# Fourier filter and two gated products in fp32r on one core: a 498-column last super-tile, the second-layer weights split by GpSimd and passed through DRAM, and a reordered first and last unit

## The reference

```python
X = np.fft.rfft(x, axis=1)
y = np.fft.irfft(X * (filt_r + 1j * filt_i)[None], n=3008, axis=1)
t = y.reshape(6016, 256)
h = t @ w_in1
t = np.where(h > 0, h, np.exp(np.minimum(h, 0)) - 1) @ w_out1
h = t @ w_in2
out = (h * np.clip(h + 3, 0, 6) / 6) @ w_out2
```

## Time and profile before

| | |
|---|---|
| median of 3 runs | 1104.79 us (1104.62 to 1105.99) |
| profiled execution | 1103.63 us, span 1101.8 us, mean granted clock 0.999 |
| PE busy | 1093.9 us, 99% of the span |
| PEld, DVE, ACT, POOL busy | 882.8, 757.3, 765.9, 280.4 us |
| DMA | 54.20 MB, 49 GB/s in the mean |

### The profile page before, as it was taken

One profiled execution on the slowest core, in us unless ns is written; L12 is line 12 of the kernel. 1 busy time (PEld: TensorE's weight loads), 2 busy tenths in 40 slices (PEclk: granted clock), 3 DMA queues, 4 the chain that ended last, 5 costly groups with the idle time before them and its releaser, 6 DMA issues.

```text
span 1101.8 us, 13377 instructions
## 1 busy us (share of the span) xinstructions
PE 1093.9 (99%) x4798; PEld 882.8 (80%) x4798; DVE 757.3 (69%) x941; ACT 765.9 (70%) x1149; POOL 280.4 (25%) x215
## 2 busy tenths in 40 slices
PE   9999999999999999999999999999999999999998
PEld 4666878888888888888887888888888888888886
DVE  7998676666666676676687866665665666666665
ACT  0554788788788788888898666566666666666654
POOL 4757051111111111120398620120121021020000
PEclk9999999999999999999999999999999999999999
DMA  9755200200100101101211201001101001000001
GB/s 288 241 173 175 91 1 3 74 1 14 63 1 31 44 1 38 39 1 38 76 58 57 76 1 38 38 1 38 38 1 38 38 1 38 38 1 1 38 1 38
DMA packets 29330, 54.20 MB, mean 49 GB/s; under 512 B 3408, under 2 KB 19664, under 8 KB 29264
## 3 DMA queue, kind: packets, MB, share of 16 engines
q1 hardware_dynamic: 23648, 44.12, 12.0%
q10 hardware_dynamic: 5616, 9.22, 2.5%
HBM read 34.83 MB, written 18.51 MB: 48 GB/s over the span
## 4 chain that ended last, share of the span: by engine, by line
PE 91%; ACT 4%; DVE 2%; issue 1%; POOL 1%; ACTq 0%; POOLq 0%
PE ps L479 43%; PE ps L470 13%; PE ps L468 13%; PE ps L469 13%; PE ps L432 3%; PE ps L400 3%; PE ps L408 2%; DVE e L776 2%; PE ps L417 1%; ACT e L634 1%; ACT w_hi L606 1%; ACT e L636 1%; PE ps L419 1%; PE ps L420 1%; PE ps L438 0%
## 5 line engine op out<-in xcount | busy, mean ns | idle before, releaser
L790 DVE TENSOR_TENSOR g_lo<-e,g_hi 128x502 fp32r<-128x502 f32 (+1 forms) x288 | 276.5, 988 | 135.0 <-ACT g_hi L669 134.3
L468 PE MATMUL ps<-op_hi,w_hi 128*128 128x502 f32 x672 | 261.9, 390 | 0.0
L470 PE MATMUL ps<-op_lo,w_hi 128*128 128x502 f32 x672 | 261.8, 390 | 0.0
L469 PE MATMUL ps<-op_hi,w_lo 128*128 128x502 f32 x672 | 261.2, 389 | 0.0
L479 PE MATMUL ps<-g_lo,w_hi 128*128 128x502 f32 x766 | 236.9, 390 | 1.2 <-DVE g_lo L790 0.9
L479 PE MATMUL ps<-g_hi,w_hi 128*128 128x502 f32 x766 | 235.7, 389 | 0.2 <-ACT g_hi L669 0.2
L479 PE MATMUL ps<-g_hi,w_lo 128*128 128x502 f32 x766 | 234.9, 388 | 0.0
L873 POOL TENSOR_TENSOR op_lo<-op_raw,op_hi 128x1004 fp32r<-128x1004 f32 (+1 forms) x48 | 100.8, 2102 | 448.3 <-ACT op_hi L614 448.1
L479 PEld LDWEIGHTS ps<-g_lo,w_hi 128*128 128x128 f32 x766 | 143.3, 188 | 32.4 <-DVE g_lo L790 3.9
L479 PEld LDWEIGHTS ps<-g_hi,w_hi 128*128 128x128 f32 x766 | 143.7, 188 | 29.9 <-ACT g_hi L669 1.2
L479 PEld LDWEIGHTS ps<-g_hi,w_lo 128*128 128x128 f32 x766 | 144.1, 188 | 29.3
(11 more groups left out here) (74 smaller groups left out, 1147.9 us busy)
## 6 DMA issues: line engine op xcount, KB each, us to landing
op_raw<-y SPq DMA_DIRECT2D x36, 251.0 KB, 3.6
x_ring<-x_dev SPq DMA_DIRECT2D x32, 192.0 KB, 4.9
y<-ystage SPq DMA_DIRECT2D x12, 502.0 KB, 2.9
out_dev<-ystage SPq DMA_DIRECT2D x11, 502.0 KB, 2.9
y<-ystage ACTq DMA_DIRECT2D x18, 235.0 KB, 2.5
f_ring<-f_dev SPq DMA_DIRECT2D x11, 384.0 KB, 6.6
w_raw<-w_dev ACTq DMA_DIRECT2D x16, 256.0 KB, 4.5
w_raw<-w_dev SPq DMA_DIRECT2D x16, 256.0 KB, 3.1
```

Of the source, the lines that this page charges most:

```text
L468: pe.matmul(out, w_hi[p][:, cols], hi, start=start, stop=False, skip_group_check=True)
L469: pe.matmul(out, w_lo[p][:, cols], hi, start=False, stop=False, skip_group_check=True)
L470: pe.matmul(out, w_hi[p][:, cols], lo, start=False, stop=True, skip_group_check=True).then_inc(done, 1)
L790: return dve.tensor_tensor(g_lo[:, tiles, :], e[:, tiles, :], f32(g_hi[:, tiles, :]), ALU.subtract)
```

## The change

- The last super-tile of each layer is 498 columns wide (`width`), so no token is made up, and the store of zeros is gone.
- The first x group is loaded by the ACT queue, ahead of `sign` and the filter; SP loads A, x group 1, BX, x group 2. The third warm-up product is 256 columns wide.
- In unit 0 the wait for `back` and the product that starts BANK_C come behind the first product up.
- ACT casts neither the eighth pair of layer 1 nor any of layer 2. POOL casts the eighth itself, right behind the filter part, and in the super-tiles 1 to 4 of layer 1 it splits two pairs of layer 2 each: the first behind `operand_sums`, the second behind `operand_lo`. The results go to a new SBUF buffer `w_out`, SP stores them in the DRAM array `w1_parts`, and in super-tile 5 SP loads them into `w_hi` and `w_lo` of each pair, once the last unit that uses them is done. PE waits for that load (`w1_loaded`).
- At the end block 21 comes ahead of block 22, and 22 and 12 are done together: all of o = 0, then all of o = 1 (`last_columns`). The last store is cut in two: partitions 0 to 63 by SP, 64 to 127 by the ACT queue.

```diff
-            load_x(0)
+            load_x(1)
             sp.dma_start(mat("BX"), mats_dev[:, P:2 * P]).then_inc(mat_loaded["BX"], 16)
-            load_x(1)
             load_x(2)
...
-            sp.wait_ge(zeroed, 2)
-            sp.dma_start(y0[:, :, TOK:].rearrange("o p t -> p o t"), pad_zero[:]).then_inc(pad_stored, 16)
...
+                for p in next_weights(s):
+                    load_w(PAIRS + p)
+                for p in next_weights(s):
+                    sp.wait_ge(w_hi_done, PAIRS + p + 1)
+                    sp.dma_start(w1_parts[p, 0], f32(w_out[:, 0, :])).then_inc(w1_hi_stored, 16)
+                    sp.wait_ge(w_lo_done, PAIRS + p + 1)
+                    sp.dma_start(w1_parts[p, 1], f32(w_out[:, 1, :])).then_inc(w1_lo_stored, 16)
                 if s == NS - 1:
+                    sp.wait_ge(w1_hi_stored, 16 * PAIRS)
+                    sp.wait_ge(w1_lo_stored, 16 * PAIRS)
                     for p in range(PAIRS):
-                        load_w(PAIRS + p)
+                        sp.wait_ge(d12_done, (NS - 1) * PAIRS + p + 1)
+                        sp.dma_start(f32(w_hi[p][:]), w1_parts[p, 0]).then_inc(w1_loaded[p], 16)
+                        sp.dma_start(f32(w_lo[p][:]), w1_parts[p, 1]).then_inc(w1_loaded[p], 16)
...
+            def last_columns(n):
...
+                pe.wait_ge(lopair, NU)
+                pe.wait_ge(lo12, NU)
+                for o in range(DH):
+                    for fi, tile in ((1, TILE22), (0, TILE12)):
...
+                    last.then_inc(last_half if o == 0 else d12_done, 1)
...
-                    pe.wait_ge(back_ready, NG - 1)
-                    for b in (BANK_B, BANK_C):
-                        pe.matmul(bank(b), w_hi[0][:, 0:P], op_hi[0][:, 0, :], start=True, stop=True)
+                    pe.matmul(bank(BANK_B), w_hi[0][:, 0:P], op_hi[0][:, 0, :], start=True, stop=True)
...
                     if u == 0:
+                        pe.wait_ge(back_ready, NG - 1)
+                        pe.matmul(bank(BANK_C), w_hi[0][:, 0:P], op_hi[0][:, 0, :], start=True, stop=True)
                         part_i(LAST_I)
...
-                if u == LATE_UNIT:
-                    weight_hi(LATE_PAIR)
-                k = u - 2 - (NS - 1) * PAIRS
-                if 0 <= k < PAIRS:
-                    weight_hi(PAIRS + k)
...
             def weight_lo(k):
+                hi, lo = (w_hi[k], w_lo[k]) if k < PAIRS else (w_out[:, 0], w_out[:, 1])
+                half = WCOL // 2
+                if k >= LATE_PAIR:
+                    pool.wait_ge(w_sum, 4 * (k + 1))
...
+                    pool.tensor_copy(hi[:, 0:half], w_raw[:, k % 2, P:P + half]).then_inc(w_half, 1)
+                    pool.tensor_copy(hi[:, half:], w_raw[:, k % 2, P + half:]).then_inc(w_hi_done, 1)
...
-                if s != NS - 1:
...
-                else:
-                    for k in range(PAIRS):
-                        weight_sums(PAIRS + k)
-                        if 1 <= k <= NOP:
-                            operand_lo(s + 1, k - 1)
-                        weight_lo(PAIRS + k)
+                later = next_weights(s)
+                if later:
+                    weight_sums(PAIRS + later[0])
+                    weight_lo(PAIRS + later[0])
+                for piece in range(NOP if s + 1 < 2 * NS else 0):
+                    operand_lo(s + 1, piece)
+                if later:
+                    weight_sums(PAIRS + later[1])
+                    weight_lo(PAIRS + later[1])
```

More of the change, by code:

```diff
@@ L215, in build @@
         w_sum, w_hi_done, w_lo_done = sem("w_sum"), sem("w_hi_done"), sem("w_lo_done")
+        w_half = sem("w_half")
+        w1_hi_stored, w1_lo_stored = sem("w1_hi_stored"), sem("w1_lo_stored")
+        w1_loaded = [sem(f"w1_loaded{p}") for p in range(PAIRS)]
         xr_loaded, t_sum = sem("xr_loaded"), sem("t_sum")
@@ L288, in load_step, with width, next_weights @@
             return p + 1 if p < 2 else w_step(p) - 3
+        def width(s):
+            return LAST_T if s % NS == NS - 1 else T
+        def next_weights(s):
+            return (2 * s - 2, 2 * s - 1) if 1 <= s <= PAIRS // 2 else ()
         def w_step(p):
@@ L436, in _ @@
             pe.wait_ge(zeroed, 1)
-            for _ in range(3):
-                pe.matmul(ps[:, 0, :], back[:, 0, 0, :], back[:, 0, 0:4, :].rearrange("p j d -> p (j d)"),
-                          start=True, stop=True)
+            for cols in (4, 4, 2):
+                pe.matmul(ps[:, 0, 0:cols * P], back[:, 0, 0, :],
+                          back[:, 0, 0:cols, :].rearrange("p j d -> p (j d)"), start=True, stop=True)
             pe.wait_ge(mat_loaded["A"], 16)
@@ L473, in down @@
             def down(v, fi, t, hi_ready, lo_ready, start, stop, done):
[L474 removed]
+                p, tile, n = v % PAIRS, 2 * fi + t, width(v // PAIRS)
                 def add(w, g, first, final):
@@ L483, in down @@
                 pe.wait_ge(hi_ready, v + 1)
-                if v == NU - 1 and done is d12_done:
-                    pe.wait_ge(lo_ready, v + 1)
-                    for o in range(DH):
-                        at = (7 + 2 * fi + o) * P
-                        cols = slice(at, at + P)
-                        pe.matmul(out_bank(o, t), w_hi[p][:, cols], g_hi[:, tile, :], start=False, stop=False,
-                                  skip_group_check=True)
-                        pe.matmul(out_bank(o, t), w_lo[p][:, cols], g_hi[:, tile, :], start=False, stop=False,
-                                  skip_group_check=True)
-                        last = pe.matmul(out_bank(o, t), w_hi[p][:, cols], g_lo[:, tile, :], start=False, stop=True,
-                                         skip_group_check=True)
-                        last.then_inc(last_half if o == 0 else d12_done, 1)
-                    return
                 add(w_hi, g_hi, start and p == 0, False)
@@ L500, in down @@
                 add(w_hi, g_lo, False, stop and p == PAIRS - 1).then_inc(done, 1)
-            for u in range(NU + 1):
+            def last_columns(n):
+                p = PAIRS - 1
+                pe.wait_ge(lopair, NU)
+                pe.wait_ge(lo12, NU)
+                for o in range(DH):
+                    for fi, tile in ((1, TILE22), (0, TILE12)):
+                        at = (7 + 2 * fi + o) * P
+                        cols = slice(at, at + P)
+                        pe.matmul(out_bank(o, 1)[:, 0:n], w_hi[p][:, cols], g_hi[:, tile, 0:n],
+                                  start=False, stop=False, skip_group_check=True)
+                        pe.matmul(out_bank(o, 1)[:, 0:n], w_lo[p][:, cols], g_hi[:, tile, 0:n],
+                                  start=False, stop=False, skip_group_check=True)
+                        last = pe.matmul(out_bank(o, 1)[:, 0:n], w_hi[p][:, cols], g_lo[:, tile, 0:n],
+                                         start=False, stop=fi == 0, skip_group_check=True)
+                    last.then_inc(last_half if o == 0 else d12_done, 1)
+            for u in range(NU):
                 v = u - 1
```

97 lines of the change are left out of this document (53 added, 44 removed).

## The result

The changed kernel takes **1106.48 us**, the median of 22 runs (1105.08 to 1109.56), against 1104.47 us for the kernel before in 22 runs: a ratio of 1.002, interval 1.0014 to 1.0027. It is 0.2% slower. That execution had a mean granted clock of 1.000; 13 of the 22 had 0.997 or 0.998, and their median is 1106.99, that of the other nine 1105.76. The experiments come back to this.

A forecast was written before the change was run, and what follows sets the result against it. PE, busy 99% of the span, was taken as the bound. Terms -0.5 -0.3 -1.9 -1.6 -1.2 -1.45 +0.1 +1.6 summed to -5.3: 1098.3 us profiled, median 1099.5, range 1097.2 to 1101.8.

The forecast's parts named there:

- so the changed order of loads costs nothing as long as it stays so: Start: reordered loads cost nothing as PE was busy 22.96 of 23.00 us; with shorter warm-up the start gains 0.5 us.
- Seam: Between filter part and unit 0: products moved ahead of the wait for `back` let `part_i` begin 0.3 us earlier.
- Pair 7: Units 3 to 5: its cast and subtraction leave them for the seam, returning the whole 1.9 us lost.
- Change of layer: Units 43 to 48: no weight splits left there, so 1.6 us comes back, with the new loads hidden.
- Width: 16 units of 498 columns instead of 502: 2880 fewer columns at 2.4 GHz, 1.2 us gained.
- The end: After the last products: earlier stores and a split last store landing in 2.2 us finish 1.45 us sooner.
- lo12: Unit 95: second L790 result, now wanted 12 matmuls before PE's end, arrives close to need; costs 0.1 us.
- Moved splits: Super-tiles 1 to 4: eight layer-2 weight splits done by POOL alone hold up DVE and cost PE 1.6 us.
- B: Rival, super-tiles 1 to 4: the moved splits cost nothing, 1097.9 us; chance 0.20.
- E: Rival, 498-wide units: the narrower width gives nothing, 1100.7 us; chance 0.12.
- C: Rival, super-tiles 1 to 4: each one's second split costs a full 0.88 us stop, 1101.4 us; chance 0.15.
- D: Rival, super-tiles 1 to 4: every moved split costs 1.93 us as pair 7 did, 1113.3 us, slower; chance 0.03.

The follow-up runs named there:

- b_shift: The kernel before with pad_zero allocated behind h2, so the later buffers lie 64 bytes lower; 1110.33 us, ratio 1.0053 to the kernel before.
- a_both: The changed kernel with a spare 64-byte tensor where pad_zero was and x group 0 loaded by SP in the old order; 1099.96 us.
- s_rows: a_both with every operand row (op, g, e, h2) at a stride of 512 elements instead of 502; 1099.41 us.
- s_plus64: a_both with 128 spare bytes instead of 64, so op1 and all behind it lie 64 bytes higher than before; 1103.43 us.
- s_whole: a_both with the last half stored by SP alone in one transfer of 128 partitions instead of two of 64; 1098.76 us.
- t_e: s_whole with 64 spare bytes between g_lo and e, so only e, h2 and w_out move up; 1099.31 us.
- a_pad: The changed kernel with a spare 64-byte tensor where pad_zero was; 1101.21 us, ratio 0.9974 to the kernel before.
- t_quarter: s_whole with GpSimd's casts and subtractions of a weight split in four pieces of 352 columns instead of two of 704; 1099.50 us.
- u_late: t_quarter with the ACT queue's first two weight loads one column group later; 1097.91 us.
- a_x0: The changed kernel with x group 0 loaded by SP again in the old order; 1102.80 us, ratio 0.9985 to the kernel before.
- s_op1: The changed kernel with x group 0 loaded by SP and 64 spare bytes between op1_lo and g_hi, so only op1 stays low; 1101.81 us.
- u_act: t_quarter with x group 0 on the ACT queue again, as in the changed kernel; 1101.09 us.

## Why the prediction was wrong, point by point

Two steps failed, and each was worth about half of the 7.4 us.

- **The step that failed first is one that isn't in it:** "Nothing that DVE, ACT or POOL do shows in those", and the pace of 10.187 and 10.22 was taken as given. The changed kernel allocates 64 bytes less ahead of op1, and its pace is another one. The order of instructions, the operations and the trace of before can't show this. The sum needed a term of unknown sign for every buffer that PE reads from a new address. In the kernel before it was worth 5.8 us (b_shift). In the changed kernel, whose 498-wide units escape it, it comes by the paces to about 4 x 0.85 for the odd super-tiles and 5 x 0.15 for the even ones, 4.2 us, against a forecast gain of 5.3. With 0.5 that the width didn't give and 1.4 that the moved splits didn't cost, that is the 3.4 us missing in units 1 to 94.
- **"so the changed order of loads costs nothing as long as it stays so"** is the second. It rested on PE's 22.96 busy of 23.00 us, which says how much PE waited, not how much room was left. The same row's DMA share of 1.04 was a sign that a load moved back might be paid. The start came out at +2.92 up to the last group, against -0.5: PE stopped three times, 3.1 us in all, and in 13 of 22 executions the mean granted clock was lower as well. The warm-up did what was said, and group 0 began 1.15 sooner; how much of that is the warm-up is uncertain, since group 0 begins at 5.33 to 5.97 us in the twelve kernels with the short one and at 6.23 in b_shift, with the long one. The gain ended at group 5. Even with the order restored, group 31 begins between 98.49 and 100.83, around the 99.44 of before: of the 0.5 nothing certain is left.
- **Seam, -0.3:** from group 31 to unit 1, 18.63 instead of 18.85: -0.2. Right.
- **Pair 7, -1.9:** 30.73 instead of 32.59. Right. POOL's casts took 0.78 each there.
- **Change of layer, -1.6:** 60.84 instead of 62.76, -1.9, of which 0.3 is the width. Right, and PE waited for no `w1_loaded`.
- **Width, -1.2:** 10.133 against 10.187 in a_both, from the third unit of a 498-wide super-tile on, 12 x 0.054 = 0.65. The mechanism is there, at about half the size, in the addresses of before; s_rows and s_plus64 show that with other addresses it can be nothing.
- **The end, -1.45:** from unit 95 to the end 0.8 less with the split store, 1.4 less with the whole one. The term was right for a whole store, which landed in 2.0; the landing of 2.2 for the halves was 2.4 and 2.7. The Trainium skill, "SBUF — State Buffer", § "Can I just issue two DMAs to hit both halves?", says that two transfers on the two halves serialize, at +6% over a single one, and that only one transfer over all 128 partitions reaches all ports. The prediction took this for "as long as the whole", and its 0.6 has no working. The trace agrees with the section's preference for the whole: 2.0 against 2.7 us.
- **lo12, +0.1:** the first L518 began 0.12 us late, at 1097.23, with g_lo there at 1097.09. Right.
- **Moved splits, +1.6:** in the units of super-tiles 1 to 4, above their pace, together 0.2 us in the changed kernel, and with the old addresses 0.8 (a_both), 1.1 (s_whole, t_e) and 1.7 (a_pad). The mechanism is that of the earlier trace rows, and 1.6 was too much everywhere but in a_pad. The gaps of 0.2 to 0.5 that were to show in four to eight units were all but absent in the changed kernel itself. The cast was to lengthen DVE's operations to near 2.4. In the unit of s_whole shown L799 took 1.64, and it was the second cast that stretched, to 1.75 from the 0.78 that one takes alone. DVE lost more beside the subtractions: over 190 to 520 us the mean of the 1004-wide L816 is 1.41 us in the changed kernel against 1.21 for L790 before, that of L802 1.27 against 1.21 for L776. The Trainium skill, "SBUF — State Buffer", § "Who interferes with whom", says that the one that starts second is held; the cast that began behind L799 agrees with it. That the lengthening could "only be placed" was the prediction's own conclusion, and it doesn't hold: with shorter pieces it shrinks, and PE's stops go.
- **The rivals.** B was nearest for the splits. E was right in other layouts. C and D didn't occur. None of them was the one that decided, and the range held no room for it: it was built from the costs of the steps alone.
- **Luck.** That a_both, at 1098.38, meets the sum's 1098.3 in its profile isn't proof of the terms. The width gave some 0.5 less than its term and the end 0.6 less, and the splits cost 0.8 less than theirs; the start, at 117.13 against 118.29, gained 0.4 more. These four cancel.

## What to carry to other kernels

When an edit adds, removes or resizes a buffer, compare the pace of an undisturbed unit before anything else; if it differs everywhere, put the old addresses back with a spare tensor and measure again before judging the edit. Where the DMA share is at its full in a stretch, take no order of loads for free, even if no engine waits there; and look at the granted clock of every execution, since the profiled one may be of the kind that kept it. It can pay to cut a long GpSimd instruction that runs beside two-input VectorE work, and not to cut a small last store in two. s_whole, t_quarter and u_late, at 1098.8, 1099.5 and 1097.9 us, beat both kernels.

## What the runs showed of the hardware that was not expected

- 64 bytes in the address of what TensorE reads change the distance between matmuls from 226.4 to 228.7 ns (10.187 and 10.293 / 45), with no wait in the record; between layouts a unit of the same 45 matmuls took 10.16 to 10.29 us. The one shift tried of tensors that PE doesn't read (t_e) had no such effect. The rule behind it stays open.
- In the changed kernel, a_x0 and b_shift the even super-tiles take 10.225 and 10.255 in turn. The turn isn't tied to a weight pair: in layer 1 of the changed kernel the longer ones are the odd units, in layer 2 the even. It is gone in s_op1, where g_hi and g_lo are back at their place; why it is there wasn't tried.
- A stop of PE of 1.81 us at the start was followed by a spell at the lower clock in one profile (0.59 in the mean of 20 to 24 us, u_act), and one of 2.38 us in another (the changed kernel) was not.
- GpSimd casts 128x704 in 0.78 us undisturbed, where its subtraction of the same shape takes 1.69.
- Two stores of 64 partitions and 127 KB on two queues landed 2.4 and 2.7 us after a common issue, one of 128 partitions and 255 KB 2.0.
